# Attention in place over batches, the first expert's split off GpSimd, and no more casting DMAs: one change to a fused attention and mixture-of-experts kernel

## The chip, the core and the metric

The kernel runs on one core of a Trainium2 chip. The metric is the device time of one execution in microseconds (us); less is better. The core has TensorE (PE) for matrix products, VectorE (DVE) and ScalarE (ACT) for elementwise work on SBUF and PSUM, GpSimd (POOL) for work on SBUF and for its DMA queue (gathers and casting transfers), and SyncE (SP), which here does nothing but issue DMAs. Each engine runs its own list of instructions in order, and waits on semaphores.

## The reference, cut to what matters

```python
# attention: B=4 batches, H=8 heads, S=576 rows, D=64, causal window of 64
scores = q @ k.T / 8; mask = (rel >= 0) & (rel < 64)
attn = exp(scores - max) / (sum + 1e-9);  x = attn @ v            # x: 2304 x 512
# experts: E=8, 512 -> 1024 -> 512, two of them for each row
noisy = x @ w_gate + log1p(exp(x @ w_noise)) * noise
top2, softmax over the two;  y = sum_k w_k * (relu(x @ w1[e_k]) @ w2[e_k])
# dense part: 512 -> 2048 -> 512
h = y @ w_in;  g = h if h >= 1, 0 if h <= -1, else (h + 1)**2 / 4;  out = g @ w_out
```

## The kernel before, in words

**Attention** works in 36 steps, one for 64 rows of one batch (all 8 heads). Before, the order is batch by batch, nine blocks each. A step's parts are spread over iterations of PE's list: iteration g does the scores of step g (L851 the mask, L855 four products), the transposes of step g-2's probabilities (L865), the products with the values of g-3 (L881), the transposes of x of g-4 (L889) and the routing logits of g-5 (L902). DVE does the row maxima (L621), the exponent's bias (L624), the copy of the transposed probabilities (L629), and the sums and the scaled x of step g-3 (L633, L635, L641; it increments `x_ready`). ACT does the exponentials (L485) and copies the transposed x (L493) and the logits (L499, L510). SP loads the queries three blocks at a time (L237, in a ring of three chunks), the keys (L241), the values (L245), and stores x (L260); its list holds, for each step, a wait on `pv_done`, the load of values, and a wait on `x_ready` before the two stores.

**Routing** is a chain of small DVE operations (L675 to L743), two products on PE, and ends in `token_of`, the list of rows for each tile of 128 slots.

**Experts.** There are 43 tiles; with these inputs 41 hold rows (5 for each of seven experts, 6 for the last), so expert 2 begins at tile 10. POOL gathers each tile's rows from HBM (L436) through four buffers; SP writes each back in sorted order (L283), and ACT fetches it (L532). Every product is made of three: weights and rows are each split in a high part of the type fp32r and a low part, the rest. PE's tile step (L968 to L985) first waits until the expert's weights are split. There are two slots of weights in SBUF: expert e uses slot e % 2. Each MB of weights comes four times over 128 x 2048 values: before, POOL issues a plain DMA into `stage` and a DMA that casts into `Wh` (L355), and then makes the low part `Wl = stage - Wh` (L345). POOL's list is: the split of expert 0 during attention, half of expert 1's during routing, eight gathers, the rest of expert 1, 35 gathers, and then experts 2 to 7, `w_in` and `w_out` in turn. Each waits until the expert that used the slot is done.

**Dense part.** Nine groups of 256 rows. The two expert outputs of each row are gathered by POOL (L461), mixed on DVE (L783, L787), transposed on PE (L1017), and go through `w_in` (L1030 to L1032) and `w_out` (L1043 to L1045). Before, the first pairs are gathered once all 43 tiles are stored.

Of the kernel before, what the change touches and what calls it, by code (L numbers as in the profile page):

```python
# [31 lines left out]
STAGE1_CONSTANTS, ALL_CONSTANTS = 13, 24  # L32
ROUTE_NEGABS, ROUTE_PICKED, ROUTE_GAP = 1, 16, 17
# [6 lines left out]

def build(nc, qT, kT, vW, noise, w_gate, w_noise, w1, w2, w_in, w_out, out):
    B, _, BLOCKS, JQ = qT.shape
# [5 lines left out]
    N = B * BLOCKS * Q  # L48
# [6 lines left out]
    SLOTS = TILES * P  # L55
    WCOLS = KD * FF + KF * D
    STG = WCOLS // 4
    GT = 256
# [6 lines left out]
    assert BLOCKS % CH == 0 and Q == 64 and D == 512 and KD * FF2 == WCOLS and FC * D == WCOLS  # L65
# [5 lines left out]
    with ExitStack() as ctx:  # L71
# [25 lines left out]
        steps128 = sb("steps128", [P, E, NT])  # L97
# [5 lines left out]
        io_p = sb("io_p", [P, 1])  # L103


        with ExitStack() as s1:
            sb = sb_in(s1)
            q_bd = sb("q_bd", [P, CH, CH, J, 2, Q])
            k_ch = sb("k_ch", [P, CH, CH + 1, JQ])
            v_win = sb("v_win", [P, CH, D])  # L110
            probs = sb("probs", [P, CH, JQ * 2])
            probsT = sb("probsT", [P, J * P])
            x_blk = sb("x_blk", [P, CH, JQ])
            xT_blk = sb("xT_blk", [P, 2, P])
            negmax = sb("negmax", [P, BLOCKS, J])
            bias = sb("bias", [P, BLOCKS, J])
            rowsum = sb("rowsum", [P, BLOCKS, J])
            rowsum_g = sb("rowsum_g", [P, BLOCKS, J])
            rowinv = sb("rowinv", [P, BLOCKS, J])
            lg = sb("lg", [P, G, 2 * E])  # L120
            mask_first = sb("mask_first", [P, P], BF16)
            mask_band = sb("mask_band", [P, P], BF16)
            ident_b = sb("ident_b", [P, P], BF16)
            w_gn = sb("w_gn", [P, KD, 2 * E])

# [45 lines left out]
        with ExitStack() as s4:  # L171
            sb = sb_in(s4)
            y_a = sb("y_a", [P, TPG, D])
# [3 lines left out]
            square = sb("square", [P, 2, 2 * GT])  # L177
            gT_h = sb("gT_h", [P, FC, GT], F32R)
            gT_l = sb("gT_l", [P, FC, GT], F32R)
            o_out = sb("o_out", [P, 2, D])  # L180
# [14 lines left out]
        q_loaded = [sem(f"q_loaded{c}") for c in range(CH)]  # L195
        k_loaded = [sem(f"k_loaded{c}") for c in range(CH)]
        v_loaded = [sem(f"v_loaded{c}") for c in range(CH)]
# [5 lines left out]
        logits_done, logits_kept = sem("logits_done"), sem("logits_kept")  # L203
# [886 lines left out]
```

## Time and profile before

| | us |
|---|---|
| median of 3 runs | 1156.21 (1152.89 to 1161.58) |
| the profiled execution | 1152.84 |
| its span in the trace | 1151.2 |
| PE busy in the span | 1088.2 (95%) |
| attention, up to the first routing operation on DVE | 0 to 151.25 |
| routing, up to the first gather | 151.25 to 183.87 |
| experts, up to the end of the last product | 183.87 to 729.3 |
| dense part | 729.3 to 1151.2 |

The stages follow one another: each begins on data that the stage ahead of it has finished. An engine's busy share says nothing of which stage it is short in; that is read from the waits in each. All times below are from the start of the span.

### The profile page before, as it was taken

To read this page: it belongs to the slowest core of one execution; us is meant where nothing else is said; L and a number is where in the kernel's file an instruction comes from. 1 tells how busy PE (TensorE), PEld (TensorE's weight loads), DVE (VectorE), ACT (ScalarE), POOL (GpSimd) and SP (SyncE) were. 2 spreads that over 40 slices of the span, in tenths; PEclk is the share of its full clock that TensorE was granted. 3 is DMA by queue.
4 is the path that set the end of the run, shared out by engine and by line. 5 is a ranking of instruction groups with operands and counts; after the bars stand their busy time and mean duration, and the time that the engine had idled before them with its cause. 6 is when DMAs were issued, how large, how long until landed. Compare 5 with 4: busy or idle time off the path is not lost.

```text
span 1151.2 us, 20087 instructions
## 1 busy us (share of the span) xinstructions
PE 1088.2 (95%) x6753; PEld 932.0 (81%) x6754; DVE 364.5 (32%) x641; ACT 347.3 (30%) x812; POOL 323.3 (28%) x228
## 2 busy tenths in 40 slices
PE   7988927999999999999999999799999999999998
PEld 5777825888788888888888888499899898998997
DVE  5587763221211221221221221242341331422421
ACT  4443530221222222222222221053252352442431
POOL 2033044534456261717061610281101101101000
PEclk9997966999999999999999999899999999999999
DMA  9996864788976553537383730542101101011000
GB/s 230 290 268 211 268 199 139 222 269 257 340 255 216 187 205 120 201 123 230 114 269 109 261 112 19 161 150 57 46 9 55 46 9 55 23 32 55 0 19 19
DMA packets 88252, 168.29 MB, mean 146 GB/s; under 512 B 29280, under 2 KB 33888, under 8 KB 87200
## 3 DMA queue, kind: packets, MB, share of 16 engines
q0 software_dynamic: 32176, 104.61, 28.4%
q1 hardware_dynamic: 43952, 41.28, 12.5%
q10 hardware_dynamic: 12096, 22.03, 5.7%
q8 instruction: 18, 0.29, 0.1%
q14 instruction: 10, 0.08, 0.0%
HBM read 135.90 MB, written 31.98 MB: 146 GB/s over the span
## 4 chain that ended last, share of the span: by engine, by line
PE 79%; DMA 10%; SPq 3%; DVE 3%; issue 2%; POOL 2%; ACT 0%; POOLq 0%; DVEq 0%; ACTq 0%
PE bank L1045 6%; PE bank L1031 6%; PE bank L1044 6%; PE bank L1030 6%; PE bank L1043 6%; PE bank L1032 6%; PE bank L983 5%; PE bank L985 5%; PE bank L984 5%; PE bank L968 5%; PE bank L970 5%; PE bank L969 5%; DMA x_sorted<-gath 5%; DMA gath<-x_rows,token_of 3%; PE bank L991 3%
## 5 line engine op out<-in xcount | busy, mean ns | idle before, releaser
L345 POOL TENSOR_TENSOR Wl<-stage,Wh 128x2048 fp32r<-128x2048 f32 x40 | 184.2, 4605 | 77.9 <-DMA Wh<-w 57.4
L1030 PE MATMUL bank<-zT_h,Wh 128*128 128x256 f32 x576 | 160.0, 278 | 0.0
L1031 PE MATMUL bank<-zT_l,Wh 128*128 128x256 f32 x576 | 159.6, 277 | 0.0
L1032 PE MATMUL bank<-zT_h,Wl 128*128 128x256 f32 x576 | 159.5, 277 | 0.0
L758 DVE COPY y_out<-bank 128x512 f32<-128x512 f32 x43 | 29.7, 692 | 368.2 <-PE bank L985 368.2
L968 PE MATMUL bank<-Wh,xT_h 128*128 x344 | 140.2, 407 | 4.7 <-DVE xT_l L749 2.0
L983 PE MATMUL bank<-Wh,hT_h 128*128 x344 | 135.5, 394 | 0.1
L970 PE MATMUL bank<-Wh,xT_l 128*128 x344 | 135.6, 394 | 0.0
L985 PE MATMUL bank<-Wh,hT_l 128*128 x344 | 135.0, 392 | 0.0
L969 PE MATMUL bank<-Wl,xT_h 128*128 x344 | 134.7, 392 | 0.0
L984 PE MATMUL bank<-Wl,hT_h 128*128 x344 | 133.6, 388 | 0.0
L550 ACT ACTIVATE hT_h<-bank 128x512 fp32r<-128x512 f32 x86 | 46.9, 596 | 260.4 <-PE bank L991 260.4
L806 DVE SCALAR_TENSOR_TENSOR bank<-bank,square 128x512 f32<-128x512 f32 x72 | 50.4, 700 | 211.1 <-ACT square L590 211.1
L1045 PE MATMUL bank<-Wh,gT_l 128*128 128x512 f32 x288 | 113.3, 393 | 0.0
L1043 PE MATMUL bank<-Wh,gT_h 128*128 128x512 f32 x288 | 113.1, 393 | 0.0
L1044 PE MATMUL bank<-Wl,gT_h 128*128 128x512 f32 x288 | 112.5, 391 | 0.0
L1030 PEld LDWEIGHTS bank<-zT_h,Wh 128*128 128x128 f32 x576 | 108.7, 189 | 0.6 <-issue 0.3
L1031 PEld LDWEIGHTS bank<-zT_l,Wh 128*128 128x128 f32 x576 | 108.7, 189 | 0.5
L1032 PEld LDWEIGHTS bank<-zT_h,Wl 128*128 128x128 f32 x576 | 108.7, 189 | 0.0
L461 POOL DMA_INDIRECT y_a<-y_sorted,pair_slot x18 | 17.1, 953 | 313.1 <-PE bank L1017 244.3
L543 ACT ACTIVATE hid<-bank 128x512 f32<-128x512 f32 x86 | 51.5, 599 | 153.0 <-PE bank L970 153.0
L968 PEld LDWEIGHTS bank<-Wh,xT_h 128*128 128x128 f32 x344 | 65.3, 190 | 17.1 <-issue 5.4
(148 smaller groups left out, 1648.5 us busy)
## 6 DMA issues: line engine op xcount, KB each, us to landing
stage<-w POOLq DMA_DIRECT2D x32, 1024.0 KB, 5.8
Wh<-w POOLq DMA_DIRECT2D x32, 1024.0 KB, 10.5
x_sorted<-gath SPq DMA_DIRECT2D x43, 256.0 KB, 3.9
y_sorted<-y_out ACTq DMA_DIRECT2D x43, 256.0 KB, 3.0
x_in<-x_sorted ACTq DMA_DIRECT2D x41, 256.0 KB, 4.4
v_win<-vW SPq DMA_DIRECT2D x36, 256.0 KB, 5.3
k_ch<-kT SPq DMA_DIRECT2D x12, 512.0 KB, 6.6
q_bd<-qT SPq DMA_DIRECT2D x24, 192.0 KB, 5.5
```

Source lines behind the costliest of these rows:

```text
L345: nc.gpsimd.tensor_tensor(Wl[:, s, cols], stage[:, c % 2], Wh[:, s, cols], ALU.subtract).then_inc(w_ready, 1)
L968: nc.tensor.matmul(H_ps[a][:], xT_h[:, u, k], high, start=(k == 0), stop=False)
L969: nc.tensor.matmul(H_ps[a][:], xT_h[:, u, k], low, start=False, stop=False)
L970: mm = nc.tensor.matmul(H_ps[a][:], xT_l[:, u, k], high, start=False, stop=(k == KD - 1))
L983: nc.tensor.matmul(Y_ps[:], hT_h[:, k], high, start=(k == 0), stop=False)
L984: nc.tensor.matmul(Y_ps[:], hT_h[:, k], low, start=False, stop=False)
L985: mm = nc.tensor.matmul(Y_ps[:], hT_l[:, k], high, start=False, stop=(k == KF - 1))
L1030: nc.tensor.matmul(here, high, zT_h[:, k], start=(k == 0), stop=False)
L1031: nc.tensor.matmul(here, high, zT_l[:, k], start=False, stop=False)
L1032: mm = nc.tensor.matmul(here, low, zT_h[:, k], start=False, stop=(k == KD - 1))
L1043: nc.tensor.matmul(O_ps[u][:], gT_h[:, k, rows], Wh[:, 1, cols], start=(k == 0), stop=False)
L1045: mm = nc.tensor.matmul(O_ps[u][:], gT_l[:, k, rows], Wh[:, 1, cols], start=False, stop=(k == FC - 1))
```

## The change

- Attention goes block by block, with the four batches in turn inside a block; the lists are written out in full. `q_bd` holds two block rows of queries (one being used, one being loaded), `k_ring` four block rows of keys, `v_ring` two, all loaded once. In SP's list the queries of row i+1 are loaded at step 4i, behind step 4i-1's wait on `x_ready` and its store. The first row is loaded in pieces, keys and values of it from ACT's queue. x is stored for two steps at a time.
- The logits of two steps are one product of 128 rows, kept in PSUM to the end; DVE's routing reads them there (one more DVE operation, two ACT copies fewer).
- Expert 0's weights are split in 16 pieces of 128 x 512, on ACT (high part) and DVE (low part), at every second attention step. POOL only issues the loads.
- All other weights: no casting DMA; POOL copies `stage` into `Wh` and then subtracts (`parts`). Expert 1's two halves come behind gathers 6 and 12.
- The first two tiles' rows of the dense part are gathered once the 41 tiles with rows are stored, and mixed on POOL; seven tiles' worth of `y_sorted` are filled with zeros before. The next two pairs are gathered, and then `w_out` is split, once all tiles are done. The 16 products that keep PE busy there go.
- Masks, the noise's layout, and the order of rows in `x_rows` are changed to fit.

```diff
+                    sp.dma_start(q_bd[rows, r % 2, :, :, hi].rearrange("p b j q -> p (b j) q"),
+                                 qT[r, rows].rearrange("p b (j q) -> p (b j) q", j=J)).then_inc(q_loaded[r % 2], 16)
+
+            def load_k(r):
+                sp.dma_start(k_ring[:, k_slot(r)], kT[r]).then_inc(k_loaded[r % 4], 16)
+
+            def load_v(b, r):
+                half = slice(64 * (r % 2), 64 * (r % 2) + 64)
+                sp.dma_start(v_ring[half, b], vW[b, Q * r:Q * r + Q]).then_inc(v_loaded[b], 16)
...
+            def step(s):
+                i, b = s // B, s % B
+
+                if b == 0 and i >= 1:
+                    sp.wait_ge(scored, s)
+                    if i + 1 < BLOCKS:
+                        load_q(i + 1)
+                    if i >= 2 and i + 2 < BLOCKS:
+                        load_k(i + 2)
+                if i >= 1 and i + 1 < BLOCKS:
+                    sp.wait_ge(pv_done, s + 1)
+                    load_v(b, i + 1)
+                if s % 2:
+                    sp.wait_ge(x_ready, s + 1)
+                    store_x(s // 2)
...
+            load_q(1)
+            load_k(2)
+            load_k(3)
...
+            for s in range(G):
+                step(s)
...
-            def low_part(n, s, c):
-
-                pool.wait_ge(w_cast[c // 2], 32 * n + 32)
-                pool.wait_ge(staged[c % 2], 32 * n + 16 * (c // 2) + 16)
+            def parts(n, s, c):
+
+                hold(staged[c % 2], 32 * n + 16 * (c // 2) + 16)
                 cols = slice(STG * c, STG * c + STG)
+                nc.gpsimd.tensor_copy(Wh[:, s, cols], stage[:, c % 2]).then_inc(high_ready, 1)
+                pool.wait_ge(high_ready, 4 * n - 4 + c + 1)
                 nc.gpsimd.tensor_tensor(Wl[:, s, cols], stage[:, c % 2], Wh[:, s, cols],
                                         ALU.subtract).then_inc(w_ready, 1)
 
...
-            fetch_first(0, [(scored, 1), (scored, 4)])
-            load_first(0, 0, 0, [(scored, k) for k in (7, 10, 14, 18, 22, 26)])
-            load_rest(0, 0)
-            fetch_first(1, [(scored, 29), (scored, 32)])
-            load_first(1, 1, 1, [(scored, 34)] + [(x_ready, G)] * 5)
+            fetch_first(0, [(scored, 3), (scored, 6)])
+            for c in range(2):
+                load_raw(0, c + 2, (w_ready, c + 1))
+            fetch_first(1, [(w_ready, 3), (w_ready, 4)])
...
-                if t == 8:
-                    load_rest(1, 1)
+                if t == 6:
+                    first_parts(1, 1, 1)
+                if t == 12:
+                    last_parts(1, 1)
...
-            pool.wait_ge(y_done, TILES + 1)
...
+            def mix_first(t):
+
+                pool.wait_ge(y_a_back[t], 16)
+                nc.gpsimd.tensor_scalar(y_a[:, t], y_a[:, t], share[:, 0, t:t + 1], None,
+                                        ALU.mult).then_inc(scaled, 1)
+                pool.wait_ge(y_b_back[t], 16)
+                nc.gpsimd.tensor_scalar(y_b[:, t], y_b[:, t], share[:, 1, t:t + 1], None,
+                                        ALU.mult).then_inc(y_b_scaled, 1)
+                pool.wait_ge(scaled, t + 1)
+                pool.wait_ge(y_b_scaled, t + 1)
+                nc.gpsimd.tensor_tensor(y_a[:, t], y_a[:, t], y_b[:, t], ALU.add).then_inc(mixed, 1)
+
+            used = pool.value_load(last_tile[0:1, E - 1:E], min_val=1, max_val=TILES + 1)
+            hold(y_kept, used)
             for t in range(TPG):
                 gather_pairs(t)
-            load_first("out", E + 1, 1)
-            load_rest(E + 1, 1)
-            for t in range(TPG, NT):
-
+            for t in range(TPG):
+                mix_first(t)
+            def next_pairs(t):
                 pool.wait_ge(zTp_done, t - TPG + 1)
                 gather_pairs(t)
 
+            for t in range(TPG, 2 * TPG):
+                next_pairs(t)
+            pool.wait_ge(y_done, TILES + 1)
...
+            def cast_piece(k):
+
+                c, cols = k // PIECES, slice(PC * (k % PIECES), PC * (k % PIECES) + PC)
+                act.wait_ge(staged[c % 2], 16 * (c // 2) + 16)
+                nc.scalar.activation(Wh[:, 0, PC * k:PC * k + PC], stage[:, c % 2, cols], ACT.Copy).then_inc(piece_cast, 1)
...
+                if s >= 4 and s % 2 == 0 and s < 4 + 8 * PIECES:
+                    cast_piece((s - 4) // 2)
...
+            def low_piece(k):
+
+                c, cols = k // PIECES, slice(PC * (k % PIECES), PC * (k % PIECES) + PC)
+                dve.wait_ge(piece_cast, k + 1)
+                inst = nc.vector.tensor_tensor(Wl[:, 0, PC * k:PC * k + PC], stage[:, c % 2, cols],
+                                               Wh[:, 0, PC * k:PC * k + PC], ALU.subtract)
+                if k % PIECES == PIECES - 1:
+                    inst.then_inc(w_ready, 1)
...
+            def scores(s):
+                i, b = s // B, s % B
+                if i == 0:
+                    pe.wait_ge(row0_loaded[b], 48)
+                elif b == 0:
+                    pe.wait_ge(q_loaded[i % 2], 32 * ((i + 1) // 2))
+                    if i >= 2:
+                        pe.wait_ge(k_loaded[i % 4], 16 * ((i + 2) // 4 if i % 4 >= 2 else i // 4))
+                if s in (0, B):
+                    pe.wait_ge(zeroed, 2 * i + 2)
+                if s == B:
...
+            for s in range(G + 5):
+                if s < G:
+                    scores(s)
+                if 2 <= s < G + 2:
+                    transposed_probs(s - 2)
+                if 3 <= s < G + 3:
+                    values(s - 3)
+                if 4 <= s < G + 4:
+                    transposed_x(s - 4)
+                if s >= 6 and s % 2 == 0:
+                    logits((s - 6) // 2)
...
-            for r in range(2):
-                pe.wait_ge(y_stored[r], 16 * ((TILES + 1 - r) // 2))
-            keep_busy(banks[0], 16)
```

The order of instructions at three places. SP in attention, before: one chunk of queries within two steps.

```order
L245 ISA [waits pv_done]
L245 DMA v_win<-vW 128x512
L237 ISA [waits scored]
L237 DMA q_bd<-qT 64x12x64
L237 ISA
L237 DMA q_bd<-qT 64x12x64
L241 DMA k_ch<-kT 128x1024
L260 ISA [waits x_ready]
L260 DMA x_rows<-x_blk 64x256
```

SP in attention after the change, at the turn from block row 1 to 2 (steps 7 and 8 of the list).

```order
L258 DMA v_ring<-vW 64x512 [waits pv_done] x2
L262 DMA x_rows<-x_blk 64x2x256 [waits x_ready]
L262 DMA x_rows<-x_blk 64x2x256
L250 DMA q_bd<-qT 64x16x64 [waits scored]
L250 DMA q_bd<-qT 64x16x64
L254 DMA k_ring<-kT 128x1024
L258 DMA v_ring<-vW 64x512 [waits pv_done] x2
```

The load of queries now stands behind a wait on `x_ready` and two stores, and goes into one of two buffers, where before there were three chunks.

POOL at the end of routing and in the gathers, before (35 gathers follow the last row but one).

```order
L345 TENSOR_TENSOR Wl<-stage,Wh 128x2048
L333 DMA stage<-w 128x4x512
L436 DMA gath<-x_rows,token_of 128x512 x8
L345 TENSOR_TENSOR Wl<-stage,Wh 128x2048 x2
L436 DMA gath<-x_rows,token_of 128x512 x35
```

POOL at the same place after the change (31 gathers follow).

```order
L467 DMA gath<-x_rows,token_of 128x512 x6
L376 CAST Wh<-stage 128x2048
L378 TENSOR_TENSOR Wl<-stage,Wh 128x2048
L365 DMA stage<-w 128x4x512
L467 DMA gath<-x_rows,token_of 128x512 x6
L376 CAST Wh<-stage 128x2048
L378 TENSOR_TENSOR Wl<-stage,Wh 128x2048
L467 DMA gath<-x_rows,token_of 128x512 x31
```

Between the first and the last gather there stood two subtractions; now there are four, each behind a copy.

POOL at the end of the experts, before and then after.

```order
L461 DMA y_b<-y_sorted,pair_slot 128x512
L355 DMA Wh<-w_out 128x4x512 x4
L345 TENSOR_TENSOR Wl<-stage,Wh 128x2048 [waits staged0,w1_cast]
L333 DMA stage<-w_out 128x4x512 [waits w_ready]
L345 TENSOR_TENSOR Wl<-stage,Wh 128x2048 [waits staged1,w1_cast]
```

```order
L506 TENSOR_TENSOR y_a<-y_a,y_b 128x512 [waits y_b_scaled,scaled]
L491 DMA y_a<-y_sorted,pair_slot 128x512 [waits zTp_done]
L491 DMA y_b<-y_sorted,pair_slot 128x512
L376 CAST Wh<-stage 128x2048 [waits y_done,staged0]
L378 TENSOR_TENSOR Wl<-stage,Wh 128x2048 [waits high_ready]
L365 DMA stage<-w_out 128x4x512 [waits w_ready]
```

The mix of the first rows and two more pairs of gathers now stand ahead of the split of `w_out`, and each part of it has a copy.

## Rows read from the trace of the kernel before

**Rows 1.** The page, part 4: the chain that ended last, by engine.

```profile
PE 79%; DMA 10%; SPq 3%; DVE 3%; issue 2%; POOL 2%; ACT 0%; POOLq 0%; DVEq 0%; ACTq 0%
```

**Rows 2.** Timeline of attention, PE: start us, us, engine, line, operation; then DVE's first routing operation.

```profile
8.07 0.58 PE L851 MATMUL bank<-mask_first,ident_b 128*128 128x512 bf16 x1 [3.23 <-POOL io_hi L407]
...
119.15 0.10 PEld L851 LDWEIGHTS bank<-mask_band,ident_b 128*128 128x128 bf16 x1
...
122.36 0.10 PEld L851 LDWEIGHTS bank<-mask_band,ident_b 128*128 128x128 bf16 x1
...
141.63 0.42 PEld L865 LDWEIGHTS bank<-ident,probs 128*128 128x128 f32 x4
...
151.25 0.31 DVE L675 SCALAR_TENSOR_TENSOR t_a<-lg 128x144 f32<-128x144 f32 x1 [3.84 <-ACT lg L499]
```

**Rows 3.** Timeline of SP's queue and DVE in one step; the queries' DMAs from 121 to 135 us.

```profile
120.03 1.14 SPq L260 DMA_DIRECT2D x_rows<-x_blk  x2
...
122.19 1.54 SPq L237 DMA_DIRECT2D q_bd<-qT  x2
...
122.62 0.42 DVE L641 TENSOR_TENSOR x_blk<-bank,rowinv 128x256 f32<-128x256 f32 x1
...
DMA to landing us min/median/max: 4.9/5.1/5.4
...
DMA to landing us min/median/max: 3.6/5.5/8.9
```

**Rows 4.** Timeline around one of POOL's subtractions in attention, and a stretch behind it.

```profile
82.31 4.51 POOL L345 TENSOR_TENSOR Wl<-stage,Wh 128x2048 fp32r<-128x2048 f32 x1
...
87.59 0.63 PE L865 MATMUL bank<-ident,probs 128*128 128x128 f32 x4 [3.18 <-DVE probsT L629]
...
90.69 0.10 PEld L851 LDWEIGHTS bank<-mask_band,ident_b 128*128 128x128 bf16 x1
...
95.91 0.10 PEld L851 LDWEIGHTS bank<-mask_band,ident_b 128*128 128x128 bf16 x1
...
90.00:92.00 2.00, 2.00 (x14) 1.87 (x14) 0.65 (x3) 1.01 (x6) 0.00 (x0) 0.50 0.69 178
```

**Rows 5.** Timeline of routing: DVE's two long operations, and the first gather.

```profile
155.02 4.57 DVE L684 TENSOR_TENSOR t_a<-noisy,top 128x144 f32<-128x144 f32 x1
...
160.31 5.20 DVE L687 TENSOR_TENSOR oh<-desc,code 128x144 f32<-128x144 f32 x1
...
183.87 1.05 POOL L436 DMA_INDIRECT gath<-x_rows,token_of  x1 [17.15 <-DVE token_of L731]
```

**Rows 6.** POOL: its one copy, gathers and subtraction; PE's wait at tile 10; stage loads.

```profile
2.04 0.29 POOL L379 CAST ident_b<-ident 128x128 bf16<-128x128 f32 x1
...
193.66 0.94 POOL L436 DMA_INDIRECT gath<-x_rows,token_of  x1 [1.25 <-DMA x_sorted<-gath]
...
207.51 0.96 POOL L436 DMA_INDIRECT gath<-x_rows,token_of  x1 [0.81 <-POOL Wl L345]
...
217.09 0.95 POOL L436 DMA_INDIRECT gath<-x_rows,token_of  x1 [1.08 <-DMA x_sorted<-gath]
...
285.63 0.95 POOL L436 DMA_INDIRECT gath<-x_rows,token_of  x1 [0.30 <-issue]
...
310.48 0.78 POOL L333 DMA_DIRECT2D stage<-w  x1 [0.67 <-POOL Wl L345]
311.27 4.58 POOL L345 TENSOR_TENSOR Wl<-stage,Wh 128x2048 fp32r<-128x2048 f32 x1
...
316.09 0.50 PE L968 MATMUL bank<-Wh,xT_h 128*128 x1 [1.62 <-POOL Wl L345]
...
stage<-w POOLq DMA_DIRECT2D x32, 1024.0 KB, 5.8
```

**Rows 7.** The turn to the dense part: DVE behind the last product, the first product with `w_in`.

```profile
729.28 0.69 DVE L758 COPY y_out<-bank 128x512 f32<-128x512 f32 x1 [5.48 <-PE bank L985]
...
744.32 0.78 PE L1030 MATMUL bank<-zT_h,Wh 128*128 128x256 f32 x1
```

More of the change, by code:

```diff
@@ L281, in bounce @@
+            for s in range(G):
+                step(s)
+            sp.wait_ge(const_ready, ALL_CONSTANTS)
+            for t in range(SURE, TILES):
+                sp.dma_start(y_sorted[P * t:P * t + P], zeros[:]).then_inc(y_cleared, 16)
             def bounce(t, r, before):
@@ L297, in _, with keep @@
             confirm((TILES - 1) % 4, 16 * ((TILES - 1) // 4) + 16)
+            def keep(u, count):
+                sp.wait_ge(y_stored[u], count)
+                sp.sem_inc(y_kept, 1)
+            sp.sem_inc(y_kept, 1)
+            with sp.Fori(0, TILES // 2) as m:
+                for u in range(2):
+                    keep(u, 16 * m + 16)
+            if TILES % 2:
+                keep(0, 16 * (TILES // 2) + 16)
             with sp.Fori(0, GROUPS) as g:
@@ L502, in _ @@
[L502 to L511 removed]
+                if s >= 5 and s % 2:
+                    t = (s - 5) // 2
+                    act.wait_ge(xT_done, s - 3)
+                    if t:
+                        act.wait_ge(logits_done, t)
+                    nc.scalar.activation(xT_blk[:].rearrange("p a h u q -> p (a h u q)"), XT_ps[:],
+                                         ACT.Copy).then_inc(xT_copied, 1)
@@ L641, in step @@
                     nc.vector.tensor_tensor(
[L642 removed]
+                        x_blk[:, t % CH, u].rearrange("p (j d) -> p j d", j=J),
                         X_ps[k % 2][:, 0:JQ].rearrange("p (j d) -> p j d", j=J),
[L644 to L650 removed]
@@ L651, in _ @@
-            for i in range(3):
-                step(B, i)
+                        rowinv[:, k % 2].unsqueeze(2).to_broadcast([P, J, Q]), ALU.mult).then_inc(x_ready, 1)
+                if s >= 5 and s % 2 and s < 5 + 8 * PIECES:
+                    low_piece((s - 5) // 2)
+            for s in range(G + 3):
+                step(s)
             n = [0]
@@ L817, in _ @@
             for u in range(TPG):
-                mix(u, u, 0)
-            for u in range(TPG):
                 low_z(u, u)
@@ new lines, in transposed_probs, with values @@
+            def transposed_probs(s):
+                pe.wait_ge(exp_done, s + 1)
+                if s >= 1:
+                    pe.wait_ge(pT_copied, s)
+                for j in range(J):
+                    mm = nc.tensor.transpose(PT_ps[:, P * j:P * j + P], probs[:, s % CH, P * j:P * j + P], ident[:])
+                mm.then_inc(pT_done, 1)
+            def values(s):
+                i, b = s // B, s % B
+                pe.wait_ge(pT_copied, s + 1)
+                pe.wait_ge(v_loaded[b], 16 * max(i, 1))
+                if s >= 2:
+                    pe.wait_ge(x_ready, s - 1)
+                for j in range(J):
+                    for hi in range(2):
+                        head = slice(P * j + Q * hi, P * j + Q * hi + Q)
+                        mm = nc.tensor.matmul(X_ps[s % 2][Q * hi:Q * hi + Q, Q * j:Q * j + Q], probsT[:, head],
+                                              v_ring[:, b, head], start=True, stop=True)
+                mm.then_inc(pv_done, 1)
```

407 lines of the change are left out of this document (172 added, 235 removed).

## The prediction

> **What bounds the kernel now.** I read the chain that ended last first. PE has 79% of it, DMAs 10% [rows 1]: nearly all is PE at its own pace, and a change pays only where the chain leaves PE. Then I read the timeline stage by stage for such places.
>
> In attention the weight loads of PE stand back to back: one iteration's scores begin at 119.15, the next at 122.36 [rows 2], 3.20 us a step. DVE and ACT have gaps in it. From the first scores at 8.07, 36 such steps would end at 123.3; the first iteration without scores begins at 141.63, so 18.4 us are lost. Part of it is the four subtractions of POOL: in one, DVE's next operation stands still, PE waits 3.18 us for DVE, and then runs at a granted clock of 0.50, its lower level of 1.2 GHz, where the step from 90.69 to 95.91 takes 5.2 us and not 3.2 [rows 4]. The rest is in the first 45 us, where loads queue. From 141.63 to the first routing operation at 151.25 there are 9.6 us more [rows 2].
>
> Routing is a chain on DVE of 32.6 us. Two of its operations take 4.57 and 5.20 us where one of the same size takes 0.31 [rows 2, 5]; POOL is subtracting beside both.
>
> The experts are PE's, but for one place: tile 10, the first of expert 2, waits 1.62 us for POOL's second subtraction, begun at 311.27 [rows 6]. Followed back, POOL does nothing from 183.87 on but gathers, subtractions and waits for DMAs. So POOL's list between the first gather and 316.09 is on the path, and each us added to it is paid, less nothing.
>
> At the turn to the dense part PE's first real product comes 15.0 us after the last one of the experts [rows 7].
>
> **The change, part by part.** The sum is made on the profiled execution, 1152.84 us with a span of 1151.2; the median of the three runs is 3.4 us above it.
>
> *Attention without new waits.* POOL subtracts nothing there, and less is loaded (keys and values once). The smaller first pieces can be in by about 6 us (estimate; 8.07 before, bounds 5 and 8). Logits in pairs halve the number of products; of 3.20 us I take off 0.15 (bounds 0 and 0.3). The casts of 16 pieces go in ACT's gaps and the subtractions in DVE's; both wait for PE once a step, so I cost them at nothing; if the first piece's load is late, ACT and everything behind it wait once, 0 to 4 us. Then 6 + 36 x 3.05 + 9.6 - 0.3 (the logit copies on ACT go) = 125.1 against 151.25, **-26**.
>
> *The new wait for queries.* SP's list loads the queries of row i+1 behind the wait on `x_ready` for step 4i-1 and its two stores. x of that step is made in DVE's part of iteration 4i+2, which ends 0.68 us into the next: 122.62 + 0.42 against 122.36 [rows 3]. Counted from the beginning T of iteration 4i+3: x ready at 0.68, stores issued from 0.87 to 2.01 (the trace has 0.19 between DVE's end and SP, and 1.14 for two), the second of two query loads issued from about 2.8 (1.54 for two) [rows 3]. From its issue to landing a load took 5.1 us in a stretch like this one [rows 3], with 192 KB where it is 256 now. So the queries are there at T + 7.9, and iteration 4i+4 wants them at T + 3.05: PE waits **4.9 us in each of seven rows** (2 to 8; row 1 is loaded ahead), 34 us. Nothing hides it: every engine works for PE's next scores, and a buffer for a row more isn't there. Bounds: 3.4 us with the fastest load of all, 3.6 [rows 3]; 6.2 with the larger load in proportion to its size. After 3.18 us of waiting the clock fell [rows 4], so I add the price of a step at the lower clock, 2 us, to each (bounds 0 and 3): 14 us. Together **+48** (bounds 24 and 64). Behind SP's late loads stand its loads of keys and values, which have a row to spare.
>
> By the Trainium skill, DMA: Bandwidth & Descriptors, Anatomy of one DMA, a DMA costs some 2.0 us and its bytes at 436 GB/s; that would be 3.2 us for both halves (an estimate), less than any such load in the trace took, and PE would wait 2.3 us a row; the sum would be 32 us less than with mine.
>
> *Routing.* The two long operations fall to 0.31: -9.77 + 0.62 = -9.15, and the new one of the same size adds 0.34: **-9**. ACT's two large broadcasts are done long before they are wanted.
>
> *POOL up to tile 10.* The first six gathers end at 194.6 as before, seen from 183.87 [rows 6]. A copy of 128 x 2048 isn't in the trace. A copy of 128 columns takes 0.29; in proportion that is 4.6 us, as much as the subtraction with two operands, 4.58. Half of that, for one operand, is 2.3 [rows 6]. I take 2.4, nearest the row of the same width, with 1.8 and 3.3 for the range. Then: two times (copy 2.4, subtraction 4.6, some 2.1 for holds and the load's issue: 0.67 and 0.78 in the row, the rest semaphores) = 18.1; six gathers, 207.51 to 218.0 = 10.5; two times (copy, subtraction, 0.65) and 0.8 = 16.1; 31 gathers, which is 207.51 to 286.6 less four at the later pace of 2.3 us = 69.9 [rows 6]. End at 309.2, where before it was 286.6. Then the loads of `stage`, 0.4 + 5.8 [rows 6], two copies and two subtractions with 2.9 between: PE begins tile 10 at about 332.3, not at 316.1: **+16** (bounds 12 and 24). The casting DMAs that vanish are worth 10 us of this already: with them the loads would land later. PE has then waited 18 us, so it begins at the lower clock: +2. The next experts have 61 us for some 31 of POOL's work, as before, and stay hidden.
>
> By the Trainium skill, GPSIMD Engine Reference, section 3.1, a body with up to two operations is bound by its port at 1.03 cycles an element; no copy of this size is in the trace. With a copy of 1.8 us by that (an estimate), tile 10 would begin 3.6 us earlier and the turn would be 2.4 us shorter.
>
> *The turn.* Tile 40, the last with rows, ends two tiles before the last product; 43 tiles take some 530 us, so that is 24 us, in which its store, four gathers and six operations on 128 x 512 fit (some 18 us, an estimate). Behind the last product stand only the transposes, their two halves, and the start: 3.4 us for 15.0, **-11.6** [rows 7]. But `w_out` is now split late: POOL issues four gathers of 0.95 and 0.30 us first [rows 6], then has four times (copy, subtraction, holds and loads), so the fourth part is ready some 39.5 us behind the last product. A group takes (1151.2 - 744.3) / 9 = 45.2 us, half of it for each matrix, so PE wants the first part at 3.4 + 22 = 25.4 and, with a quarter of a half pass, 2.7 us, between parts, the fourth at 33.5. It waits 1 us for the third part and 5 for the fourth: +6 (bounds 4 and 12). Together **-5** with something for the clock. Before, PE came later, and the same split was ready in time.
>
> *Nothing:* the zeros (SP and the queues idle in routing), the stores of x, the tables.
>
> **Sum:** -26 + 48 - 9 + 18 - 5 = +26; 1152.84 + 26 = 1179, and I say **1180**. Its own range is 1158 to 1203.
>
> **The rivals.**
>
> *The queries come in time* (SP's wait is met earlier than I count, or loads land at once). Speaks for it: before, no such load was ever waited for. Against: before there were three buffers and loads ran rows ahead. Then -26 - 9 + 18 - 5 = -22: **1131**, faster. Chance 0.13.
>
> *Short waits at full clock.* Loads at 3.6 us or less; PE waits up to 3.4 us a row, and the clock holds, as it did over some shorter gaps: +24 or less for +48: **1146 to 1155**. The skill's rule above points here. Chance 0.14.
>
> *POOL isn't late.* If copies take 1.8 us and the gathers run faster with no casting DMA beside them, tile 10 waits some 5 us and not 18: **1166**. Against: no such DMA ran beside the gathers from 207 to 287 before either. Chance 0.12.
>
> *Neither:* **1117**, chance 0.04.
>
> *Slower still,* as one mechanism: the wait for queries grows as the larger loads, stores and expert 0's stage loads share the DMA engines, 9 us a row with the clock low for most of it. It decides from about 6 us of landing time. **1205**, chance 0.09.
>
> The forecast has 0.48. A measurement of this kernel tells a change from about 1% on, 11.6 us. Faster: the first and fourth rival and a little of the second, 0.19. Within 1%: most of the second, half of the third, a little of the forecast: 0.20. Slower: 0.61. For 8 in 10 the range goes from 1140 to 1204.
>
> **What will show it.** Right: in attention PE waits for a DMA of `q_bd` seven times, some 5 us each, twelve to fourteen us of work between them, with the granted clock at 0.50 behind each; no POOL subtraction there; routing takes some 24 us; PE waits once for `Wl` at tile 10, near 17 us, and twice for parts of `w_out` in the first dense group. Wrong: PE's waits in attention are few or name ACT (the pieces' loads), or POOL's copy takes as long as its subtraction, or the gathers run at another pace than 2.3 us.

## The result, and the profile after

The changed kernel takes **1196.76 us** (median of four runs, 1192.72 to 1201.16), the one before 1156.65 in the same comparison (1152.89 to 1161.58): ratio 1.0348, 95% interval 1.0306 to 1.0391. The profiled execution took 1197.74 us with a span of 1196.2, 45.0 more than the span before. I read it in the order of the prediction.

The page, parts 1 and 4: busy time of each engine, and the chain that ended last.

```profile
PE 1106.0 (92%) x6593; PEld 944.3 (79%) x6594; DVE 348.4 (29%) x652; ACT 351.9 (29%) x797; POOL 355.4 (30%) x230
...
PE 74%; DMA 12%; issue 5%; POOL 4%; DVE 3%; SPq 2%; ACT 0%; POOLq 0%; DVEq 0%
```

DMAs and POOL have gained against [rows 1]. But PE also has fewer products than in the kernel before (6593, where its page has 6753) and is busy for longer, 1106.0 us where it has 1088.2. Steps at a lower clock make products longer too, but in attention PE's busy time grows by 2.2 us only (131.2 to 133.4); 15.5 of the 17.8 come from tile 10 on. That is the first hint of something that I had not reckoned with.

**Attention.** PE's products with the mask, the first of each row of scores (in brackets the idle time before them and what ended it), then SP's queue, the operation of DVE that it waits for, and a table by stretches of 4 us (engines' busy time, granted clock, DMA share, GB/s).

```profile
34.12 0.61 PE L913 MATMUL bank<-mask_even,ident_b 128*128 128x512 bf16 x1 [3.94 <-DMA q_bd<-qT]
55.89 0.61 PE L913 MATMUL bank<-mask_odd,ident_b 128*128 128x512 bf16 x1 [5.68 <-DMA q_bd<-qT]
75.61 0.61 PE L913 MATMUL bank<-mask_even,ident_b 128*128 128x512 bf16 x1 [5.89 <-DMA q_bd<-qT]
95.40 0.61 PE L913 MATMUL bank<-mask_odd,ident_b 128*128 128x512 bf16 x1 [5.59 <-DMA q_bd<-qT]
...
101.60 0.59 PE L913 MATMUL bank<-mask_odd,ident_b 128*128 128x512 bf16 x1
...
116.66 0.61 PE L913 MATMUL bank<-mask_even,ident_b 128*128 128x512 bf16 x1 [5.09 <-DMA q_bd<-qT]
135.86 0.61 PE L913 MATMUL bank<-mask_odd,ident_b 128*128 128x512 bf16 x1 [5.05 <-DMA q_bd<-qT]
154.07 0.61 PE L913 MATMUL bank<-mask_even,ident_b 128*128 128x512 bf16 x1 [4.96 <-DMA q_bd<-qT]
```

```profile
87.47 0.42 DVE L705 TENSOR_TENSOR x_blk<-bank,rowinv 128x256 f32<-128x256 f32 x1
87.92 2.15 SPq L262 DMA_DIRECT2D x_rows<-x_blk  x2
90.11 1.35 SPq L250 DMA_DIRECT2D q_bd<-qT  x2
```

```profile
92.00:96.00 4.00, 0.60 (x2) 0.51 (x3) 0.00 (x0) 0.00 (x0) 0.65 (x1) 0.79 1.16 262
96.00:100.00 4.00, 4.00 (x31) 3.55 (x30) 1.12 (x3) 1.32 (x8) 0.00 (x0) 0.50 0.82 273
100.00:104.00 4.00, 4.00 (x21) 3.91 (x20) 1.17 (x5) 0.70 (x3) 0.00 (x0) 0.50 0.40 98
```

Seven waits, 36.2 us in sum. The chain behind one is the one foreseen from [rows 3]: x at 87.47 + 0.42, the stores' issues from 87.92, the queries' from 90.11, and PE goes on at 95.40. Two of its terms were off in opposite directions: the two stores took 2.15 us to issue where I had 1.14, and the second load landed 4.6 us behind its issue where I had 5.1. Then PE runs at the lower level (0.50, 1.2 GHz): the step from 95.40 takes 6.2 us.

The Trainium skill (DMA: Bandwidth & Descriptors, Anatomy of one DMA) had given 3.2 us for the loads and waits of 2.3 us, by my estimate. From the first issue at 90.11 to PE's start it is 5.3 us, and the waits are 5.2 on average: the measurement decides against that estimate. The Trainium skill gives these figures for DMAs that GpSimd issues; SyncE issues these loads, so my estimate stretched them.

**Routing.** DVE's first operation, the two that were long before, and the first gather.

```profile
178.58 0.31 DVE L736 TENSOR_SCALAR noisy<-bank 128x144 f32<-128x144 f32 x1 [3.52 <-PE bank L959]
...
182.67 0.31 DVE L746 TENSOR_TENSOR t_a<-noisy,top 128x144 f32<-128x144 f32 x1
...
183.69 0.31 DVE L749 TENSOR_TENSOR oh<-desc,code 128x144 f32<-128x144 f32 x1
...
202.39 1.06 POOL L467 DMA_INDIRECT gath<-x_rows,token_of  x1 [30.94 <-DVE token_of L793]
```

Routing begins 27.3 us later than in [rows 2] and takes 23.8 us in place of 32.6 [rows 5].

**POOL up to tile 10.** A copy and a subtraction between gathers, the last gather, the loads and the second part behind it, and PE's first product of tile 10.

```profile
213.17 1.91 POOL L376 CAST Wh<-stage 128x2048 fp32r<-128x2048 f32 x1
215.17 4.58 POOL L378 TENSOR_TENSOR Wl<-stage,Wh 128x2048 fp32r<-128x2048 f32 x1
...
327.29 0.95 POOL L467 DMA_INDIRECT gath<-x_rows,token_of  x1 [0.30 <-issue]
328.43 1.53 POOL L365 DMA_DIRECT2D stage<-w  x2 [0.18 <-issue]
337.48 1.89 POOL L376 CAST Wh<-stage 128x2048 fp32r<-128x2048 f32 x1 [7.52 <-DMA stage<-w]
...
347.38 4.49 POOL L378 TENSOR_TENSOR Wl<-stage,Wh 128x2048 fp32r<-128x2048 f32 x1
...
352.11 0.79 PE L1029 MATMUL bank<-Wh,xT_h 128*128 x1 [19.09 <-POOL Wl L378]
```

From the first gather to tile 10 it is 149.7 us, before 316.09 - 183.87 = 132.2 [rows 5, 6]: +17.5. The copy takes 1.91 us (I took 2.4), the load and its issue 9.05 (I took 6.2). Behind the wait of 19.1 us PE begins tile 10 at the lower clock:

```profile
352.00:354.00 2.00, 1.89 (x5) 1.51 (x6) 0.00 (x0) 0.00 (x0) 1.47 (x2) 0.50 0.00 0
354.00:356.00 2.00, 2.00 (x6) 1.61 (x5) 0.00 (x0) 0.00 (x0) 1.91 (x2) 0.50 0.94 264
```

The tile's `y_out` copy comes at 378.48, 26.4 us behind its first product; before it was 339.79 - 316.09 = 23.7. Some 2.5 us of this are the clock.

**The turn.** DVE's copy behind the last product of the experts, the first product with `w_in`, and PE's only wait for `w_out`.

```profile
774.40 0.69 DVE L820 COPY y_out<-bank 128x512 f32<-128x512 f32 x1 [5.58 <-PE bank L1046]
777.57 0.36 PE L1091 MATMUL bank<-zT_h,Wh 128*128 128x256 f32 x1 [1.04 <-DVE zT_l L854]
...
809.24 0.50 PE L1106 MATMUL bank<-Wh,gT_h 128*128 128x512 f32 x1 [0.25 <-POOL Wl L378]
```

3.2 us and not 15.0 [rows 7], and no wait to speak of behind it.

**What is left over.** 27.3 - 8.8 + 17.5 - 11.8 = 24.2, and 2.5 for the clock in tile 10 make 26.7, but the span grew by 45.0. The rest lies where nothing waits. ACT's copies of `o_out` end the two halves of a dense group; here one whole group, first in the changed kernel, then in the kernel before.

```profile
905.91 0.60 ACT L652 ACTIVATE o_out<-bank 128x512 f32<-128x512 f32 x1
916.57 0.60 ACT L652 ACTIVATE o_out<-bank 128x512 f32<-128x512 f32 x1 [10.06 <-PE bank L1108]
951.97 0.60 ACT L652 ACTIVATE o_out<-bank 128x512 f32<-128x512 f32 x1
```

```profile
914.13 0.61 ACT L601 ACTIVATE o_out<-bank 128x512 f32<-128x512 f32 x1
924.60 0.60 ACT L601 ACTIVATE o_out<-bank 128x512 f32<-128x512 f32 x1 [9.87 <-PE bank L1045]
958.78 0.61 ACT L601 ACTIVATE o_out<-bank 128x512 f32<-128x512 f32 x1
```

46.06 us against 44.65, with the granted clock at 1.00 in both and the same products. Two expert tiles take 25.02 us against 24.61. From tile 10 to the end of the experts it is 422.3 us against 413.2, 9.1 more, of which the clock in tile 10 was 2.5 and this pace is 6.6; in the dense part the pace is 11.7. Together 18.3, and 26.7 + 18.3 = 45.0. (The expectations below count the 2.5 as pace too and so say 20.6.)

Nothing in the code of these products had changed. What had was where their operands lie in SBUF. (In the dense part the order of the tensors had changed too, `square` and `gT` ahead of `y_a` and `zT`; a_pad32 below keeps the new order.) `steps128` is bfloat16 now, 288 bytes a partition less, and `zeros` has 2048 more: 1760 is a multiple of 32 and not of 64. All tensors of the stages (`q_bd`, `xT_h`, `hT_h`, `gT_h`, `zT_h` and the rest) begin at 32 past a multiple of 64 bytes; before, they began at a multiple of 64.

### The profile page after: what moved, and what is told of

The parts are those of the page before. It is cut to its first block, busy times and chain, and to the rows that moved or that the text cites. A ratio compares the mean times of both kernels' runs of the same rounds, so it can differ in the third digit from the quotient of the medians.

```text
span 1196.2 us, 19454 instructions
## 1 busy us (share of the span) xinstructions
PE 1106.0 (92%) x6593; PEld 944.3 (79%) x6594; DVE 348.4 (29%) x652; ACT 351.9 (29%) x797; POOL 355.4 (30%) x230
## 4 chain that ended last, share of the span: by engine, by line
PE 74%; DMA 12%; issue 5%; POOL 4%; DVE 3%; SPq 2%; ACT 0%; POOLq 0%; DVEq 0%
PE bank L1108 5%; PE bank L1107 5%; PE bank L1106 5%; PE bank L1046 5%; PE bank L1044 5%; PE bank L1045 5%; PE bank L1029 5%; PE bank L1031 5%; PE bank L1030 5%; PE bank L1092 5%; PE bank L1093 5%; PE bank L1091 5%; DMA q_bd<-qT 4%; DMA x_sorted<-gath 4%; DMA gath<-x_rows,token_of 3%
## 5 line engine op out<-in xcount | busy, mean ns | idle before, releaser
L378 POOL TENSOR_TENSOR Wl<-stage,Wh 128x2048 fp32r<-128x2048 f32 x36 | 165.9, 4608 | 3.0
L1029 PE MATMUL bank<-Wh,xT_h 128*128 x344 | 141.2, 410 | 21.2 <-POOL Wl L378 19.8
L1030 PE MATMUL bank<-Wl,xT_h 128*128 x344 | 137.1, 399 | 0.0
L376 POOL CAST Wh<-stage 128x2048 fp32r<-128x2048 f32 x36 | 68.4, 1901 | 155.3 <-PE bank L1046 141.9
```

The source lines that it names most:

```text
L1029: nc.tensor.matmul(H_ps[a][:], xT_h[:, u, k], high, start=(k == 0), stop=False)
L1030: nc.tensor.matmul(H_ps[a][:], xT_h[:, u, k], low, start=False, stop=False)
```

## The experiments

The kernel before was measured again beside each group of runs, with medians from 1156.0 to 1158.8 us. Differences of 2 or 3 us between versions of different groups are therefore not read from the medians.

### The place in SBUF: a_pad32 and b_pad32

The changed kernel and the kernel before, each with one unused tensor of 32 bytes.

```diff
+        pad = sb("pad", [P, 8])
         zeros = sb("zeros", [P, D])
```

```diff
         io_p = sb("io_p", [P, 1])
+        pad = sb("pad", [P, 8])
```

> The changed kernel with one unused tensor of 32 bytes a partition ahead of zeros, so that the SBUF tensors behind it (queries, keys, xT, hT, zT, gT and the rest) start at multiples of 64 bytes again, as in the kernel before; the edit of steps128 to BF16 had moved them to 32 past such a multiple. Theory: it is this offset that slows PE's products, 0.2335 us for 0.2287 in the experts, 46.06 us for 44.65 a dense group. Then both go back, which is 8.9 + 11.7 = 20.6 us: 1176 (1173 to 1180, more if attention's steps get shorter too). Rival: the pace comes from the instruction list or from more work beside PE; then nothing changes, 1197.

> The kernel before with the same 32 unused bytes behind io_p, so that all tensors of the stages start 32 past a multiple of 64 bytes and nothing else changes. Theory of the offset: the experts' products take 0.2335 us, a dense group 46.06, and the whole 1156.7 + 20.6 = 1177, some more if attention slows too. Rival (instruction list, other work): 1157.

Measured: the changed kernel with the pad 1177.77 us, ratio to the kernel before 1.0171 (1.0133 to 1.0209) where it was 1.0348; the kernel before with the pad 1174.63, ratio 1.0143 (1.0105 to 1.0182). ACT's copies of `o_out` over the nine dense groups, first to last start, of the changed kernel, of it with the pad, and of the kernel before with the pad:

```profile
L652 ACT ACTIVATE o_out<-bank x18: 597/599/605, 813.7 to 1192.0; 128x512 f32<-128x512 f32 x18
```

```profile
L653 ACT ACTIVATE o_out<-bank x18: 597/598/608, 799.8 to 1166.6; 128x512 f32<-128x512 f32 x18
```

```profile
L602 ACT ACTIVATE o_out<-bank x18: 597/599/606, 787.0 to 1164.6; 128x512 f32<-128x512 f32 x18
```

378.3, 366.8 and 377.6 us; the kernel before has 366.7. So 32 unused bytes take the slow pace from one kernel and give it to the other, with the rest of the code as it was: the place is the cause, and the instruction list isn't. The kernel before got 15.8 us slower by the medians, 17.7 by the profiled spans, and not 20.6 as expected; 2.5 of the 20.6 were the clock in tile 10.

### The queries' loads: a_early_q

```diff
-                if b == 0 and i >= 1:
-                    sp.wait_ge(scored, s)
-                    if i + 1 < BLOCKS:
-                        load_q(i + 1)
-                    if i >= 2 and i + 2 < BLOCKS:
-                        load_k(i + 2)
+                if b == 0 and i + 1 < BLOCKS:
+                    sp.wait_ge(scored, s + B)
+                    if i + 2 < BLOCKS:
+                        load_q(i + 2)
+                    if i >= 1 and i + 3 < BLOCKS:
+                        load_k(i + 3)
```

> The changed kernel, with SP issuing the loads of a row's queries and keys one row's step earlier in its list: behind the wait for the last scores of the row two before, and ahead of the waits and stores of the four steps that follow. Theory: the seven waits of PE for q_bd (36.2 us in sum) go, and with them the stretches at half clock behind them (some 14 us by my estimate): the first routing operation comes at some 130 us in place of 178.6, the whole is 1147 (1145 to 1161). Rival: the waits are the larger loads' own time on the DMA engines; then PE still waits some us in each row, and less than half of it comes back, 1175 or more.

Measured: 1145.42 us, ratio 0.9866 (0.9823 to 0.991). That is 51 us less than the changed kernel, and faster than the kernel before. The same table by stretches, three of PE's products with the mask, and DVE's first routing operation:

```profile
30.00:34.00 4.00, 4.00 (x19) 3.91 (x20) 0.50 (x2) 1.05 (x5) 0.00 (x0) 0.50 0.52 152
...
92.00:96.00 4.00, 4.00 (x45) 3.63 (x44) 3.05 (x10) 3.24 (x16) 0.00 (x0) 1.00 0.40 106
96.00:100.00 4.00, 4.00 (x57) 3.62 (x55) 3.32 (x9) 2.19 (x10) 0.70 (x1) 1.00 1.19 188
...
94.46 0.38 PE L913 MATMUL bank<-mask_odd,ident_b 128*128 128x512 bf16 x1
97.80 0.38 PE L913 MATMUL bank<-mask_odd,ident_b 128*128 128x512 bf16 x1
100.32 0.38 PE L913 MATMUL bank<-mask_odd,ident_b 128*128 128x512 bf16 x1
...
127.52 0.31 DVE L736 TENSOR_SCALAR noisy<-bank 128x144 f32<-128x144 f32 x1 [2.69 <-PE bank L959]
```

From 40 to 110 us PE is busy all the time and the clock stays at 1.00; steps take 3.3 and 2.5 us in turn. Routing begins 51.1 us earlier. The waits were 36.2 of it; the other 14.9 are, as far as these traces show, what the lower clock cost, net. From the first product of row 2 to routing the changed kernel takes 178.58 - 34.12 = 144.5 us, this one 127.52 - 35.8 = 91.7; less the six waits in that stretch (32.3) some 20 us are left for the steps behind the seven waits. The step from 95.40 took 6.2 where it takes 3.3 at full clock. Against this, a_early_q is at row 2 5.6 us later than the changed kernel would be without its first wait (30.2); its clock was 0.50 from 10 to 18 and from 30 to 34 us. What made the waits was an order in SP's list: DMAs of 1.35 us to issue stood behind a wait for x that they don't need.

### Expert 1's split off POOL: a_e1_dve

```diff
-                if t == 6:
-                    first_parts(1, 1, 1)
-                if t == 12:
-                    last_parts(1, 1)
+                if t in (12, 18):
+                    c = (t - 12) // 6
+                    load_raw(1, c + 2, (w_ready, 5 + c))
...
-            tile_step(0, 0)
+            for t in range(5):
+                tile_step(t, t % 2)
+                if t < 4:
+                    for k in range(4):
+                        cast_next(4 * t + k)
```

`cast_next(k)` copies piece k of `stage` to `Wh` on ACT; on DVE `low_next(k)` subtracts it, four pieces ahead of each of tile steps 1 to 4.

> The changed kernel with expert 1's split taken off POOL: 16 pieces of 512 columns, copied by ACT at the ends of tile steps 0 to 3 and subtracted by DVE at the beginnings of steps 1 to 4; POOL only issues the last two loads, between gathers. Theory: POOL's list between the first gather and tile 10 loses four copies of 1.9 us, four subtractions of 4.6 and their holds, some 30 us, so the wait of 19.1 us at tile 10 goes, and 2 us of low clock: 1176 (1174 to 1179). Rival: the gathers' own pace makes POOL late anyway, or the pieces hold ACT and DVE up so that PE waits in tiles 0 to 4: 1190 or more.

Measured: 1175.35 us, ratio 1.0139 (1.0104 to 1.0175), 21 less than the changed kernel. DVE's copies of `y_out`, one a tile, of the changed kernel and of this one:

```profile
L820 DVE COPY y_out<-bank x43: 691/692/693, 231.7 to 774.4; 128x512 f32<-128x512 f32 x43
```

```profile
L839 DVE COPY y_out<-bank x43: 691/692/693, 234.2 to 755.4; 128x512 f32<-128x512 f32 x43
```

542.7 and 521.2 us: the wait at tile 10 is gone, no other of note came, and the gathers' own pace isn't the limit.

### POOL's parts beside routing: a_pool_route

```diff
+            first_parts(1, 1, 1)
             pool.wait_ge(tokens_ready, 1)
...
-                if t == 6:
-                    first_parts(1, 1, 1)
```

> The changed kernel, with POOL's first two parts of expert 1 (copy and subtraction of 128x2048 each, and the loads behind them) moved ahead of the wait for the routing's result, so that they lie beside DVE's routing chain and not between the gathers. Theory: DVE operations that meet the subtraction take 4.6 us or more in place of 0.3, as two did in the kernel before, so the routing chain gets 4 to 10 us longer than 23.8; POOL's list behind the first gather gets 15 us shorter, so the wait of 19.1 us at tile 10 falls to some 4: 1197 - 15 + 7 = 1188 (1183 to 1192). Rival: DVE's two long operations in the kernel before had another cause; the routing stays at 23.8 us, 1181.

Measured: 1182.79 us, ratio 1.0202 (1.0157 to 1.0246). The wait at tile 10 is gone, and the first gather comes at 210.49, 8.1 us later, as expected in size, but not at the place expected. The total is nearer to the rival's 1181, which had the chain unharmed, and the chain was unharmed; but the rival's reason, another cause for the long operations, doesn't hold either. POOL was earlier than I had thought, and its first two operations met attention's last steps, where they cost DVE 5.3 us (the waits for queries were 2.8 us longer in this trace as well); the routing chain took 23.8 us as before. POOL and DVE there:

```profile
173.99 1.90 POOL L376 CAST Wh<-stage 128x2048 fp32r<-128x2048 f32 x1
175.98 4.51 POOL L378 TENSOR_TENSOR Wl<-stage,Wh 128x2048 fp32r<-128x2048 f32 x1
```

```profile
173.74 2.19 DVE L696 TENSOR_SCALAR rowsum_g<-rowsum 128x4 f32<-128x4 f32 x1
...
176.52 0.68 DVE L691 COPY probsT<-bank 128x512 f32<-128x512 f32 x1
177.12 3.40 DVE L696 TENSOR_SCALAR rowsum_g<-rowsum 128x4 f32<-128x4 f32 x1
...
186.67 0.31 DVE L735 TENSOR_SCALAR noisy<-bank 128x144 f32<-128x144 f32 x1 [4.72 <-PE bank L958]
```

An operation on 128x4 numbers in SBUF, elsewhere 0.16 us, takes 2.19 and 3.40, and ends when POOL's copy (175.89) and subtraction (180.49) end. The copy from PSUM between them takes its usual 0.68, and `noisy`, which reads PSUM, 0.31 beside POOL's second subtraction (183.86 to 188.36). The Trainium skill has this as a port pair that DVE and POOL share, held for a whole instruction (SBUF — State Buffer, Who interferes with whom); both ends in this trace agree.

### The turn as it was: a_late_turn

```diff
-            hold(y_kept, used)
+            hold(y_kept, TILES + 1)
```

> The changed kernel, in which POOL gathers the first pairs of the dense part only when all stores of y are done, as before the change, and not when the stores up to the last tile with rows are. Theory: the first product of w_in comes some 15 us behind the last of the experts in place of 3.2, and w_out's split moves back with the gathers: 4 x 0.95 us of gathers, then 24 us of splits, against some 26 us until PE wants the first part, so a few us more: 1196.8 + 12 to 20 = 1209 to 1217. Rival: POOL's split of w_out covers nothing of it and PE's clock falls too: 1220 or more; or the turn isn't bound by the gathers: 1198.

Measured: 1216.54 us, ratio 1.0503 (1.0459 to 1.0547), 19.8 us more. The first product of `w_in`, at 796.04, comes 20.7 us behind the copy of `y_out` at 775.3, and not 3.2. Two waits of PE for the mixing on POOL are most of it:

```profile
788.43 1.11 PE L1078 MATMUL bank<-ident,y_a 128*128 128x128 f32 x4 [13.13 <-POOL y_a L506]
792.93 1.11 PE L1078 MATMUL bank<-ident,y_a 128*128 128x128 f32 x4 [3.38 <-POOL y_a L506]
```

### The three together: a_best

The edits of a_pad32, a_early_q and a_e1_dve.

> The changed kernel with the three edits of the first four experiments together: 32 unused bytes ahead of zeros, the queries' loads a row's step earlier, expert 1's split on ACT and DVE. Theory: they act in different stretches and add up: 1196.8 less 19 (measured alone), 51 (alone), 21 (alone) = 1106; against the kernel before a ratio near 0.956. Rival: with attention 50 us shorter expert 0's and 1's weights come too late for the pieces, or one gain swallows another; then 1115 to 1130.

Measured: **1103.26 us** (1101.06 to 1106.19, six runs), ratio to the kernel before 0.954 (0.9508 to 0.9571). The gains add up within 3 us of the expected 1106, and the version beats both kernels. Of PE's waits beyond start and routing none is above 1.7 us.

### Which places are good: b_part, b_pad64, b_w64, a_best2, a_best3

The kernel before with 32 bytes ahead of `xT_h`, of `zT_h` and of `square` (b_part), with 64 behind `io_p` (b_pad64), with 64 ahead of `Wh` and of `stage` (b_w64):

```diff
+            pad3 = sb("pad3", [P, 8])
             xT_h = sb("xT_h", [P, 2, KD, P], F32R)
...
+        pad1 = sb("pad1", [P, 16])
         Wh = sb("Wh", [P, 2, WCOLS], F32R)
```

and a_best with 64 bytes ahead of `xT_h`, `gT_h` and `y_a` (a_best2); in a_best3 the last of these is 192 bytes.

> The kernel before, with xT_h, xT_l, hT_h, hT_l (operands loaded into PE's array in the experts) and zT_h, zT_l (operands streamed through it in the first half of a dense group) at 32 past a multiple of 64 bytes; square, gT_h, gT_l, o_out and all of attention at multiples of 64 again. Nothing else differs. Theory that the offset of either kind of operand counts: the 42 tiles from the first to the last y_out copy take 520 us as with all shifted (514.6 before), the product groups of w_in as much longer as there (some 1.0 us a dense group) and those of w_out nothing, so 1172. Rival A, only the streamed operand counts: 514.6 in the experts, dense part longer, 1166. Rival B, only the loaded one: experts 520, dense as before, 1163. Rival C, it is attention's, x_in's or gath's offset, neither: 1157.

> The kernel before with 64 unused bytes behind io_p: all stage tensors stay at multiples of 64 bytes but move from 64 past a multiple of 128 to a multiple of 128. Theory that 64 is the unit that counts: 1157, tiles and dense groups as before. Rival, coarser units count too: as the step from 32 to 64 gave 18 us, a step to 128 could give some more, 1140 to 1150, or, if the unit is another, lose.

> The kernel before with Wh and Wl, and nothing else, moved by 64 bytes to 64 past a multiple of 128 (all others keep their place modulo 128, zT 64 past one). With all stage tensors at multiples of 128, and Wh too, eight and a half dense groups had taken 375.3 us in place of 366.7, the products of w_in being slower. Theory A, what counts there is that the loaded operand Wh and the streamed zT begin at the same place modulo 128: w_in becomes slow here as well, 375 us, 1158.7 + 9 = 1168 or so. Theory B, zT's own place counts: 366.7 as before, and the whole moves only by what Wh as a streamed operand does in the experts and w_out, 1155 to 1162.

> The kernel with the three edits together, and 64 more unused bytes in three places, so that xT, hT and gT (the operands loaded into PE's array) begin at multiples of 128 bytes, while zT stays 64 past one. In the kernel before with everything moved by 64 bytes, a pair of expert tiles took 24.49 us in place of 24.61 and half a pass of w_out 10.36 in place of 10.47, while w_in got slower. Theory: the first two come along, the last doesn't: 21 pairs by 0.12 and 18 half passes by 0.11 are 4.5 us, 1103.3 - 4.5 = 1099. Rival: nothing, or the gain was that of one trace, 1103.

> As the kernel before this one with all edits (xT, hT, gT at multiples of 128), but zT_h and zT_l moved on by 128 bytes, from 192 to 64 past a multiple of 256, where they lie in the kernel before and in the one with three edits; gT and the rest stay. In that kernel 24.6 us of a dense group went to w_in, in the two others 23.7. Theory: zT's place modulo 256 decides; w_in goes back to 23.7 and with the faster half passes a dense group takes 44.4 to 44.5 us, the experts 24.5 a pair: 1103.3 - 4.5 = 1099. Rival: gT's place beside zT decides (gT is written while w_in's products run); w_in stays at 24.6, 1106.

Measured: b_part 1168.64 us (ratio 1.0105, 1.0059 to 1.0151); b_pad64 1162.06 (1.0033, 1.0003 to 1.0064); b_w64 1164.24 (1.0052, 1.0022 to 1.0082); a_best2 1106.42 (0.9555, 0.9525 to 0.9585); a_best3 1106.25 (0.9569, 0.9531 to 0.9608). The last two had been expected at 1099; they gained nothing on a_best. The table has where the tensors begin, in bytes past a multiple of 128, and times at full clock: of two tiles (`y_out` copies near 510), of a pass of `w_out` (between the two `o_out` copies of a group), and of `w_in` (to the next group's first copy, less a pass). Each row is from one trace, but the five kernels with the places of the changed one agree within 0.02 us in each column, and so do the three with those of the kernel before.

```
kernel           Wh   xT,hT  gT   zT    two tiles  w_out   w_in
before            0    64    64   64     24.61     10.47   23.71
a_best            0    64    64   64     24.61     10.47   23.71
changed kernel    0    32    32   32     25.02     10.66   24.74
b_pad32           0    96    96   96     24.99     10.65   24.67
b_part            0    96     0   96     25.01     10.38   24.68
b_pad64           0     0     0    0     24.49     10.37   24.98
b_w64            64    64    64   64     24.50     10.39   24.97
a_best2           0     0     0   64     24.51     10.37   24.57
a_best3           0     0     0   64     24.51     10.38   24.52
```

Two things can be read off. In the experts and in `w_out`, where `Wh` and `Wl` are streamed through PE's array, an offset of 32 or 96 costs 1.5 to 1.8%, and with the other operand at the streamed one's place modulo 128 they are fastest. In `w_in`, where `Wh` and `Wl` are loaded, the layout of the kernel before is the only fast one of those tried, and all others cost 3.4 to 5.4%. No wait is in this either: from one product to the next it is 0.113 us in the kernel before, 0.118 in a_best2, 0.119 in the changed one and 0.120 in b_pad64. Why stays open. That `zT` and `Wh` must not begin at the same place modulo 128 fits b_pad64 and b_w64, but not a_best2. `zT`'s place modulo 256 was my next theory; it fell with a_best3, which has that of the kernel before. `gT`'s place may count in a_best2 and a_best3 (there it differs from `zT`'s), but b_w64 is slow with `gT` and `zT` at 64. So a_best keeps the old places. Its median is the lowest, but by 3 us only, and the intervals of a_best2 and a_best3 overlap with its own.

## Why the prediction was right, and where not

The direction and the order of size were right: slower, 1180 with a range to 1204, measured 1196.8. Step by step:

- **Attention without new waits**: first routing operation at 125.1; with the waits taken out it came at 127.52. Right within 2.4 us, though not step by step: at full clock a step takes 2.9 us and not 3.05, and row 2 begins 5.6 us late, with the clock low ahead of it. The 32 bytes are no part of it: a_best begins routing another 4.3 us earlier, at 123.27, but all of that lies ahead of row 2 (31.4 for 35.8); from there it takes 91.9 us, and a_early_q 91.7.
- **The new wait for queries**: 4.9 us in seven rows and 14 for the clock, +48. Measured 5.2 us on average, and 51 in all by a_early_q; the lower clock cost some 20 in this kernel, 15 net. This was the largest term and the mechanism was the foreseen one: an order in a queue, read from the list and priced with three rows.
- **Routing**: -9; measured -8.8. a_pool_route shows the cause as well, though on attention's last steps and not in the chain: DVE's operations in SBUF stand while POOL's run.
- **POOL up to tile 10**: +16, measured +17.5; with the clock +18, measured 20.0, and 21 by a_e1_dve. The six copies at 1.91 us for 2.4 took some 3 us off, the load (9.05 for 6.2) put as much on.
- **The turn**: -11.6, measured -11.8. The +6 for waits on `w_out` was mis-sized: 0.2. With four copies at 1.91 and not 2.4, the fourth part was ready 34.8 us behind the last product and not 39.5, and PE's half pass with `w_in` was slower. Undoing the early gathers costs 19.8 us, more than the 11.8; PE then waits for the mixing, which is POOL's now and was DVE's.
- **"*Nothing:* the zeros, [...] the tables"**: this is the step that failed. I costed `zeros` and the bfloat16 `steps128` by the time in which they are written and read, and overlooked that they move the tensors allocated behind them. It is worth 1196.8 - 1177.8 = 19 us of the 40. Without it the changed kernel takes 1177.8, 2 us from the predicted 1180. That close hit has luck in it. By the terms of the sum, -26 was -23.7, +48 was +51.1, -9 was -8.8, +18 was +20.0 and -5 was -11.9: +26.7 where I had +26, but 7 us less at the turn cancel nearly 8 more elsewhere.

Of the rivals, "queries in time" and "short waits" fell with the seven waits of 5 us, "POOL isn't late" with the 19.1 us at tile 10, and "slower still", which had 9 us a row, with the same seven waits. The copy of 1.8 us by the Trainium skill (GPSIMD Engine Reference, section 3.1) was nearer to the measured 1.91 than my 2.4. But the load's longer time hid it, so tile 10 came no earlier.

## What to carry to other kernels

In a queue that runs in order, put a load right behind the wait that it needs, not behind waits and stores of other work: one such place cost 51 of 1197 us here, 15 of it beyond the seven waits of 5 us, by the lower clock behind them. Look at the addresses whenever a tensor is added or changes its type, even one that is touched once: with PE the bound, 32 bytes cost 19 us, and no wait in any view shows it; the time between two like events at full clock does. What a chain on POOL costs, count from its first to its last instruction, and look for engines with gaps before you add to it.

## What the runs showed of the hardware

- PE's float32 products depend on where both operands begin in SBUF: 0.41 us in 24.61 for two tiles, up to 1.27 in 23.71 for `w_in`, with the granted clock at 1.00. Which places are good isn't settled beyond the table.
- POOL's copy of 128x2048 from float32 takes 1.91 us, its subtraction of two such operands 4.6. Beside either, DVE's small operation from SBUF to SBUF stands until POOL's instruction ends (0.16 us became 2.19 and 3.40). Operations of DVE that read PSUM don't: 23 of `hT_l<-bank,hT_h` inside POOL's subtractions of the changed kernel took 0.68 to 0.69 us.
- Behind a wait of 5.6 us the granted clock was 0.50, and PE's next step took 6.2 us, which takes 3.3 at 1.00. Behind seven waits of 3.9 to 5.9 us that came to some 20 us.
